# Layer-normalised rows turned by VectorE and moved by transfers from the fifth block on, in a retention and two-layer feed-forward kernel

## What is computed

```python
def _moe2_ref(x, w_in, w_out, g_ln) -> np.ndarray:      # x: 3072 x 512, w_in: 512 x 1024, w_out: 1024 x 512
    h = x @ w_in
    h_max = np.max(h, axis=-1, keepdims=True)
    e = np.exp(h - h_max)
    sm = e / (np.sum(e, axis=-1, keepdims=True) + 1e-09)
    solu = h * sm
    mu = np.mean(solu, axis=-1, keepdims=True)
    var = np.mean((solu - mu) ** 2, axis=-1, keepdims=True)
    ln = (solu - mu) / np.sqrt(var + 1e-06) * g_ln
    return (ln @ w_out).astype(np.float32)
```

## Time and profile before

| | us |
|---|---|
| median of three runs | 982.59 |
| lowest and highest | 982.49, 983.64 |
| the profiled execution, whole | 983.99 |
| its span, from first to last instruction | 982.2 |

### The profile page before, as it was taken

The page is one execution under the profiler, slowest core; times in us unless marked ns, Lnnn a source line. Parts: engine busy times, 40 slices in busy tenths (PEclk is TensorE's granted clock), DMA queues, the critical chain, the costliest instruction groups (busy, mean ns, idle before and its releaser), DMA issues.

```text
span 982.2 us, 15207 instructions
## 1 busy us (share of the span) xinstructions
PE 958.3 (98%) x5494; PEld 849.6 (86%) x5494; DVE 616.8 (63%) x1054; ACT 548.3 (56%) x940; POOL 135.5 (14%) x170
## 2 busy tenths in 40 slices
PE   8879899999999999999999999999999999999998
PEld 4666787887899999999999999999888888888887
DVE  3777886777778653544678877677554444544442
ACT  3554645555465442433445555554687776667765
POOL 4313401102015510000151101010000000000000
PEclk9989999999999999999999999999999999999999
DMA  8747636536143513131553735521411111111100
GB/s 264 226 138 213 185 134 184 171 141 185 54 182 113 193 49 114 65 113 57 174 200 117 242 116 179 178 81 43 161 44 43 43 43 43 43 43 43 46 29 33
DMA packets 82320, 116.03 MB, mean 118 GB/s; under 512 B 7120, under 2 KB 62800, under 8 KB 82256
## 3 DMA queue, kind: packets, MB, share of 16 engines
q1 hardware_dynamic: 76800, 98.79, 30.6%
q0 software_dynamic: 4736, 15.73, 4.6%
q10 hardware_dynamic: 720, 0.66, 0.2%
HBM read 77.41 MB, written 37.75 MB: 117 GB/s over the span
## 4 chain that ended last, share of the span: by engine, by line
PE 83%; DVE 5%; issue 3%; DMA 3%; ACT 2%; POOL 2%; SPq 1%; DVEq 0%; ACTq 0%; POOLq 0%
PE psum L884 10%; PE psum L887 10%; PE psum L886 10%; PE psum L359 9%; PE psum L361 9%; PE psum L360 9%; PE psum L922 6%; PE psum L920 6%; PE psum L923 6%; PE psum L777 3%; PE psum L811 2%; PE psum L964 2%; PE psum L801 2%; PE psum L790 2%; DMA w_raw<-weights 1%
## 5 line engine op out<-in xcount | busy, mean ns | idle before, releaser
L884 PE MATMUL psum<-xo_hi,w_hi 128*128 128x384 f32 x560 | 195.3, 349 | 6.7 <-DVE psum L1494 2.6
L887 PE MATMUL psum<-xo_hi,w_lo 128*128 128x384 f32 x560 | 188.4, 336 | 0.0
L886 PE MATMUL psum<-xo_lo,w_hi 128*128 128x384 f32 x560 | 188.3, 336 | 0.0
L884 PEld LDWEIGHTS psum<-xo_hi,w_hi 128*128 128x128 f32 x560 | 105.9, 189 | 13.1 <-DVE xo_lo L1480 3.8
L886 PEld LDWEIGHTS psum<-xo_lo,w_hi 128*128 128x128 f32 x560 | 105.9, 189 | 0.8 <-issue 0.3
L1102 ACT ACTIVATE xo_hi<-b 128x768 fp32r<-128x768 f32 x84 | 70.6, 846 | 63.6 <-PE psum L923 51.9
L887 PEld LDWEIGHTS psum<-xo_hi,w_lo 128*128 128x128 f32 x560 | 105.7, 189 | 0.0
L1374 DVE TENSOR_TENSOR xo_lo<-b,xo_hi 128x768 fp32r<-128x768 f32 x84 | 80.0, 955 | 34.3 <-ACT xo_hi L1102 34.0
L359 PE MATMUL psum<-w_in_hi,x_hi 128*128 128x512 f32 x192 | 76.8, 400 | 0.3 <-ACT h_buf L1223 0.3
L361 PE MATMUL psum<-w_in_hi,x_lo 128*128 128x512 f32 x192 | 74.9, 390 | 0.0
L360 PE MATMUL psum<-w_in_lo,x_hi 128*128 128x512 f32 x192 | 74.9, 390 | 0.0
(11 more groups left out here) (128 smaller groups left out, 2065.8 us busy)
## 6 DMA issues: line engine op xcount, KB each, us to landing
act_dram<-act_buf SPq DMA_DIRECT2D x48, 384.0 KB, 2.4
b<-act_dram SPq DMA_DIRECT2D x48, 384.0 KB, 4.8
kq_buf<-k_t SPq DMA_DIRECT2D x32, 192.0 KB, 2.7
kq_buf<-q_t SPq DMA_DIRECT2D x64, 96.0 KB, 3.0
q_dec<-q_t SPq DMA_DIRECT2D x32, 192.0 KB, 2.5
w_raw<-weights POOLq DMA_DIRECT2D x12, 512.0 KB, 4.6
x_dram<-x_tile SPq DMA_DIRECT2D x4, 1536.0 KB, 6.0
x_tile<-x_dram SPq DMA_DIRECT2D x4, 1536.0 KB, 6.8
```

What stands on the lines that cost most here:

```text
L884: pe.matmul(dst, hi[:, cols], xo_hi[:, i, kc, :], start=i in (P1, P7) and kc == 0, stop=False, skip_group_check=True)
L886: pe.matmul(dst, hi[:, cols], xo_lo[:, i, kc, :], start=False, stop=False, skip_group_check=True)
L887: mm = pe.matmul(dst, lo[:, cols], xo_hi[:, i, kc, :], start=False, stop=kc == HK - 1, skip_group_check=True)
```

## The change

Tile 0 is still turned by TensorE. From tile 1 on (block 4 of 0 to 23, the fifth), `turn` is gone, and so are 20 times eight transposes. In its place:

- The mean and the deviation are now applied ahead of the product. `negative_mean` makes the mean; `square_solu` (ScalarE) squares solu plus the negative mean, and `deviation_of_pair` takes the root for two blocks at once; `invert_pair` and `normalize` (VectorE) follow.
- `turn_blocks` (VectorE) turns the normalised block in squares of 32x32, into `z0` or `z1` by the tile's parity.
- `move_turned` (SyncE) puts the squares in place, from SBUF to SBUF into `ln_t`: 16 transfers in a tile, each from 32 partitions to 32 partitions, 8 x 128 numbers on each, 128 KB. Four of them (`f`) make one group `i`. A group holds 32 rows of each of the tile's four blocks, so it needs all four blocks turned (`z_ready`, `BLOCKS * t`). `store_out` puts the rows back in their order.
- `ln_high` and `ln_low` read `ln_t` in SBUF for tiles 1 to 5, and PSUM for tile 0. `ln_high` waits for its group's four transfers.
- `scale_out` has no scale left in tiles 1 to 5.

TensorE also runs further ahead: in tile 0 it makes two `up` for each `down2`, and from tile 1 on the `up` that stands ahead of `down2` of block n is that of block n + 6. For `down2` of the last six blocks no `up` is left; there `ln_high` and `ln_low` are made a block ahead (`next_block`). The loops over tiles are written out. `solu_0` has four slots for tile 0 alone. `load_x2` and the rounding of x move with the `up`.

The diff, cut to its core. The two long lists of tile 0 (ScalarE's and VectorE's) are shown by a few lines:

```diff
+        def run_up_of(t, j):
+            tile, block = (t + 1, j + 2) if j < 2 else (t + 2, j - 2)
+            return (tile, block) if tile < C_TILES else None
+        def next_block(t, j):
+            return (t, j + 1) if j < BLOCKS - 1 else (t + 1, 0)
+        def z_of(t):
+            return z1 if t % 2 else z0
+        def ln_source(t, j, g):
+            if t == 0:
+                return psum[:, TURN[g], :]
+            return ln_t[:, j, 4 * g:4 * g + 4, :].rearrange("p k n -> p (k n)")
...
-                sp.dma_start(out[bass.ds(n * P, P), :], out_buf[:, j % 2, :]).then_inc(out_stored[j % 2], DMA)
+                if t == 0:
+                    rows = out[n * P:(n + 1) * P, :]
+                else:
+                    rows = out[bass.ds(t * TC, TC), :].rearrange("(b i c) d -> i b c d", b=BLOCKS, i=PARTS)[j]
+                sp.dma_start(rows, out_buf[:, j % 2, :]).then_inc(out_stored[j % 2], DMA)
...
+            load_x2(0, 1)
...
-            def stage_c(t, first, last):
-                if not last:
-                    sp.wait_ge(x2_lo_ready, 2 * t + 1)
-                    load_x2(0, t + 1)
-                if not first:
-                    store_out(t - 1, 3)
-                store_out(t, 0)
...
+            def move_turned(t):
+                for i in range(PARTS):
+                    sp.wait_ge(z_ready, BLOCKS * t)
+                    sp.wait_ge(ln_lo_ready, 2 * (BLOCKS * (t - 1) + i + 1))
+                    for f in range(PARTS):
+                        sp.dma_start(ln_t[32 * f:32 * f + 32, i, :, :],
+                                     z_of(t)[32 * i:32 * i + 32, :, f, :, :].rearrange("p k j c -> p k (j c)")).then_inc(
+                                         ln_t_moved[i], DMA)
+            def stage_c(t):
+                if t == 0:
...
+                    move_turned(1)
+                    return
+                if t + 2 < C_TILES:
+                    load_pair(t + 2)
+                store_out(t - 1, 3)
+                for j in range(3):
+                    if (t, j) == (C_TILES - 2, 2):
+                        move_turned(t + 1)
+                    store_out(t, j)
+                if t + 2 < C_TILES:
+                    move_turned(t + 1)
...
+            def both_up(t, j):
+                for s in range(2):
+                    up(t, j, s)
+            def stage_c(t):
+                if t == 0:
...
+                    both_up(0, 3)
+                    for j in range(1, BLOCKS):
+                        turn(0, j)
+                        both_up((2 * j + 2) // BLOCKS, (2 * j + 2) % BLOCKS)
+                        both_down2(0, j)
+                        both_up((2 * j + 3) // BLOCKS, (2 * j + 3) % BLOCKS)
+                    return
...
-                    elif not last or j < 1:
-                        turn(t, j)
-                        for s in range(2):
-                            if j < 2:
-                                up(t, j + 2, s)
-                            else:
-                                up(t + 1, j - 2, s)
-                        down2(t, j, 0)
-                        down2(t, j, 1)
-                    elif j == 1:
-                        turn(t, 1)
-                        up(t, 3, 0)
-                        up(t, 3, 1)
...
+                    if run_up_of(t, j):
+                        both_up(*run_up_of(t, j))
+                    both_down2(t, j)
...
-                act.wait_ge(turned, n * 2 + g + 1)
+                if t == 0:
+                    act.wait_ge(turned, n * 2 + g + 1)
+                else:
+                    act.wait_ge(ln_t_moved[j], DMA * PARTS * t)
                 at_least(act, y2_done, n * 2 + g - 3)
-                act.activation(ln_t_hi[:, j % 2, 4 * g:4 * g + 4, :].rearrange("p k n -> p (k n)"), psum[:, TURN[g], :],
+                act.activation(ln_t_hi[:, j % 2, 4 * g:4 * g + 4, :].rearrange("p k n -> p (k n)"), ln_source(t, j, g),
                                ACT.Copy).then_inc(ln_hi_ready, 1)
...
+            def square_solu(t, j):
+                n, one = t * BLOCKS + j, slice(j, j + 1)
+                act.wait_ge(mean_ready, n + 1)
+                at_least(act, d_squared, n - BLOCKS)
+                at_least(act, pair_std_ready, 2 * (t - 2) + j // 2 + 1)
+                act.activation(d_squares[:], solu[:, j % 2, :], ACT.Square, bias=mean[:, one],
+                               accum_out=squares_sum[:, one]).then_inc(d_squared, 1)
+            def deviation_of_pair(t, q):
+                n, pair = (t - 1) * BLOCKS + 2 * q, slice(2 * q, 2 * q + 2)
+                act.wait_ge(d_squared, n + 2)
+                act.activation(std[:, pair], squares_sum[:, pair], ACT.Sqrt,
+                               bias=eps_col[:], scale=1.0 / F2).then_inc(pair_std_ready, 1)
             def scale_out(t, j):
                 n = t * BLOCKS + j
                 act.wait_ge(y2_done, 2 * (n + 1))
-                act.wait_ge(rstd_ready, n + 1)
                 at_least(act, out_stored[j % 2], DMA * (t * (BLOCKS // 2) + j // 2))
-                act.activation(out_buf[:, j % 2, :], psum[:, Y2[j % 2], :], ACT.Copy,
-                               scale=rstd[:, j % 2:j % 2 + 1]).then_inc(out_ready, 1)
+                if t == 0:
+                    act.wait_ge(rstd_ready, n + 1)
+                    act.activation(out_buf[:, j % 2, :], psum[:, Y2[j % 2], :], ACT.Copy,
+                                   scale=rstd[:, BLOCKS + j:BLOCKS + j + 1]).then_inc(out_ready, 1)
+                else:
+                    act.activation(out_buf[:, j % 2, :], psum[:, Y2[j % 2], :], ACT.Copy).then_inc(out_ready, 1)
...
+            def stage_c(t):
+                if t == 0:
+                    copy_h(0, 2, 0)
...
+                    copy_h(2, 0, 1)
+                    square_solu(1, 3)
+                    deviation_of_pair(1, 1)
+                    deviation(0, 3)
+                    exponent(2, 0)
+                    scale_out(0, 3)
+                    copy_h(2, 1, 0)
+                    square_solu(2, 0)
...
+                    if j > 0:
+                        scale_out(t, j - 1)
+                    elif t > 1:
-                    ln_high(t, j, 0)
-                    deviation(t, j)
+                    if run_up_of(t, j):
+                        both_high(t, j)
+                    elif (t, j) != (C_TILES - 1, 3):
+                        both_high(*next_block(t, j))
+                    last_up = (t + 1, j + 1) if j < 3 else (t + 2, 0)
+                    if last_up[0] < C_TILES:
+                        square_solu(*last_up)
+                        if j % 2 == 0:
+                            deviation_of_pair(t + 1, j // 2)
+                    if run_up_of(t, j):
+                        copy_h(*run_up_of(t, j), 0)
+                        if run_up_of(t, j) == LAST_BLOCK:
+                            both_high(*next_block(t, j))
+                        if j % 2 == 1 and t + 2 < C_TILES:
+                            x2_high(t + 2, j // 2)
+                        copy_h(*run_up_of(t, j), 1)
+                        exponent(*run_up_of(t, j))
...
+            def negative_mean(t, j):
+                dve.wait_ge(solu_ready, t * BLOCKS + j + 1)
+                dve.tensor_scalar(mean[:, j:j + 1], solu_sum[:, j % 2:j % 2 + 1], -1.0 / F2, None,
+                                  ALU.mult).then_inc(mean_ready, 1)
+            def normalize(t, j):
+                dve.wait_ge(pair_rstd_ready, 2 * (t - 1) + j // 2 + 1)
+                dve.tensor_scalar(solu[:, j % 2, :], solu[:, j % 2, :], mean[:, j:j + 1], rstd[:, j:j + 1], ALU.add,
+                                  ALU.mult).then_inc(normalized, 1)
+            def turn_blocks(t, j):
+                dve.wait_ge(normalized, n - BLOCKS + 1)
+                if j == 0:
+                    for i in range(PARTS):
+                        at_least(dve, ln_t_moved[i], DMA * PARTS * (t - 2))
+                dve.transpose(z_of(t)[:, :, :, j, :].rearrange("p k f c -> p (k f) c"),
+                              solu[:, j % 2, :].rearrange("p (b r) -> p b r", r=32)).then_inc(z_ready, 1)
...
+            def invert_pair(t, q):
+                dve.wait_ge(pair_std_ready, 2 * (t - 1) + q + 1)
+                dve.reciprocal(rstd[:, 2 * q:2 * q + 2], std[:, 2 * q:2 * q + 2]).then_inc(pair_rstd_ready, 1)
...
+            def stage_c(t):
+                if t == 0:
+                    both_low(0, 0)
...
+                    take_up(1, 3)
+                    row_max(2, 0)
+                    invert_pair(1, 1)
+                    turn_up(1, 2)
+                    turn_up(1, 3)
+                    invert_deviation(0, 3)
+                    take_up(2, 0)
+                    row_max(2, 1)
+                    take_up(2, 1)
...
+                    if run_up_of(t, j):
+                        both_low(t, j)
+                    elif (t, j) != LAST_BLOCK:
+                        both_low(*next_block(t, j))
+                    if t + 1 < C_TILES:
```

(41 more changed lines are left out.)

215 lines of the change are left out of this document (147 added, 68 removed).

## The result

| | before | after |
|---|---|---|
| median, us | 982.65 (6 runs) | 978.73 (6 runs) |
| lowest and highest | 981.79, 983.64 | 977.80, 979.10 |
| the profiled execution, whole, and its span | 983.99, 982.2 | 977.80, 976.0 |
| stage C, first matmul to last | 283.3 | 274.9 |
| from the last matmul to the end | 3.6 | 7.4 |

By the medians the kernel became 3.9 us faster. The ratio is 0.9956, with an interval from 0.9942 to 0.9971, which is 4.3 us (2.8 to 5.7). The prediction had 9.1. The direction is right and the size is not. The table already says where to look: stage C became 8.4 us shorter, and behind its last matmul 3.8 us were given back. (The two spans differ by 1.5 us more than that, because stages A and B, which the change does not touch, happened to be 1.5 us shorter in the second execution: stage C's first matmul starts at 693.72 in place of 695.26.)

The account below looks back on a forecast made before the run. TensorE's row of work was taken to bound stage C. The terms -17.8 + 0.7 + 2.3 + 4.0 + 1.7 = -9.1 us, set against the median, gave 973.5 us, with 966.5 to 980.0 holding 8 in 10.

Parts of the forecast that it names:

- The period and the 17.8 us: Stage C, TensorE: the period falls from 11.79 to 10.90 us; 20 turns at 0.89 us each come off.
- Steady tiles: Steady tiles of stage C: turning adds 1.22 us to VectorE, 7.3 of 10.9 us in all, and nothing waits.
- Rivals 2 and 4: VectorE turns at 2.44 us, 979.9 us (chance 0.11); TensorE's matmul pitch rises beside the transfers, 982.6 us (chance 0.04).
- The transfers: Moves into ln_t: 0.45 us to issue each, 4.5 us from last turned block to first group landed.
- rival 3: Slow transfers set the last tile's pace; a loss once the first group takes over 7.5 us; chance 0.08.
- The end of tile 0: TensorE waits 0.7 us ahead of up(2, 2) for a copy and 2.3 us for ln_low of block 4.
- The last tile: TensorE stands still 4.0 us ahead of down2 of block 20, then loses 1.7 us to a lower clock.
- rival 1: TensorE never waits, so nearly all of the 17.8 us is gained: 964.8 to 967.5 us; chance 0.17.
- the clock's term: Behind the 4 us wait in the last tile the granted clock falls, losing 1.7 us of TensorE's work.
- Stores and x loads that have over 10 us to spare.: SyncE's queue: stores and x loads behind a tile's 16 moves, 7.2 us of issuing, can afford the delay.
- The end behind the last matmul stays as it is.: After stage C's last matmul: scale_out and the store still take 3.6 us, so no change in the sum.

Follow-up runs that it names:

- e1: The changed kernel with each store of a block's 128 result rows as four transfers of 32 rows that lie together: 973.77 us, ratio 0.9909 to the kernel before.
- e3: The changed kernel with its stores as one run of 128 rows, as before the change, so out's rows come in another order: 972.78 us, ratio 0.9896.
- e9: e1 plus e6's seventeen unread matmuls ahead of down2 of block 20: 972.16 us, ratio 0.9888 to the kernel before.
- e10: e1 plus e5's order of the last tile: 970.15 us, ratio 0.9870 to the kernel before.
- e6: The changed kernel plus seventeen matmuls whose result nobody reads, ahead of down2 of block 20: 980.41 us, ratio 0.9967 to the kernel before.
- e5: The changed kernel with only the last tile's order changed, block 22 rooted, normalised and turned before block 23's softmax: 978.15 us, ratio 0.9955 to the kernel before.

## Why the prediction was right and wrong, step by step

- **The period and the 17.8 us.** Right: 10.88 for the predicted 10.90, so 20 blocks give 20 x 0.91 = 18.2.
- **Steady tiles.** Right: the turning took 1.25 for 1.22, no wait between block 5 and block 19, VectorE busy 7.1 in 10.9 us for the predicted 7.3. Rivals 2 and 4 of the prediction fall with this.
- **The transfers.** Right in sum: from the last turned block (937.4) to the first `ln_high` (942.2) 4.8 us for 4.5, landing in 3.0. But an issue took 0.69 us, not 0.45; the six of the earlier trace rows were loads from memory of another shape. The transfers don't set the pace of blocks 21 to 23 (e1 and e3 have no wait there), and rival 3 falls.
- **The end of tile 0.** 0.7 + 2.3 were predicted; from start to start it was 0.4 ahead of up(2, 2), behind the copy of h, and 1.8 ahead of block 4. Both waits are where the prediction had them, and the chain was drawn 0.8 us too long.
- **The last tile.** 4.3 from start to start (4.05 in brackets) for 4.0, and 1.6 to 1.7 of the clock behind it for 1.7. Right, and rival 1 falls; e9 takes the clock's term away, and e10 both.
- **"Stores and x loads that have over 10 us to spare."** Wrong for one place. In the last tile the store of block 18 stands behind the 16 moves; they take 11.1 us to issue and the store 7.4 until its slot is free, and the slot is wanted before that. It cost 1.8 us from start to start ahead of block 22; e1 and e3, whose stores have other forms, have no such wait behind the same moves.
- **"The end behind the last matmul stays as it is."** Wrong: 7.4 in place of 3.6, and this is the larger part of the miss. It is the step that failed: the sum had this term at nothing, and it was 3.8. The prediction took the store's 2.0 us over to a store whose pattern the diff had changed, though the section on the change names that (`store_out` puts the rows back in their order); a row for one pattern was used for another.

The sum made again with the measured terms, in the prediction's order: -18.2 + 0.4 + 1.8 + 4.3 + 1.6 = -10.1, where it had -9.1. e3, which has the old stores, measured -10.2 by the ratio. Then the two terms that the prediction did not have: + 1.8 ahead of block 22 and + 3.8 at the end, which gives -4.5. The profiled executions have -8.4 + 3.8 = -4.6, and the ratio says -4.3. So no part of the miss stays open that the runs could tell from noise, and the form of the stores is all of it: with the old stores the kernel comes out 1.1 us faster than forecast (e3).

## What to carry to other kernels

When a layout changes so that a transfer's rows come in groups, the transfer's pattern has to be priced anew, even if its bytes are the same: a small number as its slowest dimension cost here about three times the landing time, and splitting it into plain transfers cured it for 1.7 us of issuing. Read the diff for every transfer whose pattern it alters, and look at the last one in the program first, since nothing hides it. And of several waits in a row, one that hangs on something else, as block 22's did on a store, takes back what was gained ahead of it: e6's fill gained only once that store was fast (e9), and e5's order gained most of its worth only then (e10).

## What the runs showed of the hardware

- 256 KB stored as 4 x 32 rows left SyncE waiting 5.2 to 5.3 us at the end, at 92 GB/s and a share of 0.24 of the transfer engines. As 16 x 8 rows it was 2.3, as 128 rows 1.7, and as four transfers of 32 rows 1.3 behind 1.7 of issuing.
- A store of 256 KB as 128 rows landed in 2.0 us, and in 3.9 right behind 16 transfers of 128 KB in the same queue (e3).
- Transfers of 128 KB from 32 partitions to 32 cost SyncE 0.69 us to issue in a row of 16 (11.09 us), and landed in 3.0.
- A turn of 128 x 1024 numbers in squares of 32 x 32 took VectorE 1.25 us, as long as a plain row maximum, in spite of its scattered writing.
- Filling TensorE's wait with matmuls that nobody needs held the granted clock at 1.00, and stage C was 1.5 us shorter (e9), though block 20's operands came no earlier.
- The granted clock fell to about 0.50 behind waits of 2.5, 3.1 and 4.0 us (e5, e6, the changed kernel), and stood at 1.00 behind waits of 1.1 to 1.5 us (e10, the changed kernel).
